# Context of an attention pair in three thirds of 192 queries, one beat behind the moves

## The reference

```python
scores = scale * np.matmul(q, k.transpose(0, 1, 3, 2))
thresh = np.max(scores, axis=-1, keepdims=True) - tau
scores = np.where(scores >= thresh, scores, -1000000000.0)
attn = np.exp(scores - max); attn = attn / (sum(attn) + 1e-09)
x = matmul(attn, v)                     # heads joined: 2304 x 512
h = x @ w_in;  x = (s * relu(h)**2 + b) @ w_out         # layer 0
h = x @ w_in;  x = (h * sigmoid(1.702 * h)) @ w_out     # layer 1
```

## Time and profile before

| | us |
|---|---|
| median of 3 runs (lowest to highest) | 1163.02 (1158.73 to 1167.03) |
| the profiled execution | 1155.08 |
| its span, first to last instruction | 1153.3 |
| TensorE busy | 1050.9 (91%) |
| VectorE busy | 615.6 (53%) |
| GpSimd busy | 782.8 (68%) |
| ScalarE busy | 678.0 (59%) |

### The profile page before, as it was taken

How to read it: one execution, slowest core, us unless ns; L and a number is a source line. 1 busy time by engine, 2 the same in 40 slices (tenths; PEclk the granted TensorE clock), 3 DMA queues, 4 the chain that set the end, 5 groups by cost and what they waited for, 6 DMA issues and landing times.

```text
span 1153.3 us, 18602 instructions
## 1 busy us (share of the span) xinstructions
PE 1050.9 (91%) x6144; PEld 930.8 (81%) x6144; DVE 615.6 (53%) x1556; ACT 678.0 (59%) x1267; POOL 782.8 (68%) x773
## 2 busy tenths in 40 slices
PE   4677547999999999999999999999999999999998
PEld 3565436887888878888898989989999999999997
DVE  6766859998999989897223222232222322222221
ACT  4655436766767677676467666654545545454543
POOL 4655538887878777886476666756676766766673
PEclk9889769999999999999999999999999999999999
DMA  2111177776776767855543443433444434343441
GB/s 96 42 54 53 53 186 201 188 182 178 205 208 179 189 182 198 213 156 153 152 128 117 125 124 120 128 113 125 156 128 146 130 126 155 128 150 126 147 136 65
DMA packets 126623, 162.66 MB, mean 141 GB/s; under 512 B 27328, under 2 KB 68928, under 8 KB 126528
## 3 DMA queue, kind: packets, MB, share of 16 engines
q1 hardware_dynamic: 126528, 161.47, 48.4%
HBM read 124.85 MB, written 4.72 MB: 112 GB/s over the span
## 4 chain that ended last, share of the span: by engine, by line
PE 73%; DVE 9%; SPq 8%; DMA 4%; issue 3%; POOL 2%; ACT 1%; ACTq 0%; DVEq 0%; POOLq 0%
PE y_ps L454 30%; PE scores L436 24%; SPq L282 6%; PE scores L401 5%; PE shared L436 5%; PE scores L349 5%; DVE prob L533 4%; DVE scores L509 4%; DMA prob_t<-blocks 3%; PE shared L401 2%; POOL win_lo L809 1%; SPq L291 1%; PE shared L463 1%; POOL k_lo L789 1%; PE y_ps L371 0%
## 5 line engine op out<-in xcount | busy, mean ns | idle before, releaser
L809 POOL TENSOR_TENSOR win_lo<-raw_in,win_hi 128x512 fp32r<-128x512 f32 x192 | 289.1, 1506 | 97.4 <-ACT win_hi L672 97.4
L816 POOL TENSOR_TENSOR wout_lo<-raw_out,wout_hi 128x512 fp32r<-128x512 f32 x192 | 254.9, 1328 | 100.3 <-ACT wout_hi L679 100.3
L562 DVE TENSOR_TENSOR gate<-scores,gate 128x384 f32<-128x384 f32 x134 | 74.7, 558 | 409.3 <-ACT gate L689 298.5
L454 PE MATMUL y_ps<-wout_hi,g_hi 128*128 128x512 f32 x576 | 227.7, 395 | 0.0
L454 PE MATMUL y_ps<-wout_hi,g_lo 128*128 128x512 f32 x576 | 227.2, 394 | 0.0
L454 PE MATMUL y_ps<-wout_lo,g_hi 128*128 128x512 f32 x576 | 227.2, 394 | 0.0
L640 ACT ACTIVATE prob<-scores,neg_max 128x576 f32<-128x576 f32 (+2 forms) x160 | 118.7, 742 | 144.5 <-DVE scores L509 137.7
L707 ACT CAST g_hi<-gate 128x384 fp32r<-128x384 f32 x192 | 98.6, 514 | 143.5 <-PE y_ps L454 143.2
L436 PE MATMUL scores<-act_hi,win_lo 128*128 128x384 f32 x536 | 180.9, 337 | 0.0
L436 PE MATMUL scores<-act_hi,win_hi 128*128 128x384 f32 x536 | 180.5, 337 | 0.0
L436 PE MATMUL scores<-act_lo,win_hi 128*128 128x384 f32 x536 | 180.0, 336 | 0.0
(11 more groups left out here) (66 smaller groups left out, 1668.1 us busy)
## 6 DMA issues: line engine op xcount, KB each, us to landing
raw_in<-slabs_a SPq DMA_DIRECT2D x96, 256.0 KB, 3.1
raw_out<-slabs_a SPq DMA_DIRECT2D x96, 256.0 KB, 2.8
raw_in<-slabs_b SPq DMA_DIRECT2D x96, 256.0 KB, 2.6
raw_out<-slabs_b SPq DMA_DIRECT2D x96, 256.0 KB, 2.6
qk_raw<-qk SPq DMA_DIRECT2D x32, 576.0 KB, 4.0
prob_t<-blocks SPq DMA_DIRECT2D x144, 100.0 KB, 3.1
prob_t<-blocks SPq DMA_DIRECT2D x144, 80.0 KB, 2.6
v_sb<-v SPq DMA_DIRECT2D x16, 320.0 KB, 3.2
```

What stands on the lines that cost most here:

```text
L454: mm = nc.tensor.matmul(y_ps[g][:], gp[:, n % 2, toks], wp[n % RING_OUT][:], start=(f == 0 and k == 0), stop=(f == SLABS - 1 and k == 2))
L809: nc.gpsimd.tensor_tensor(win_lo[n % RING_IN][:], raw_in[:, n % 2, :], win_hi[n % RING_IN][:].bitcast(F32), ALU.subtract).then_inc(win_lo_ ...
L816: nc.gpsimd.tensor_tensor(wout_lo[n % RING_OUT][:], raw_out[:, n % 2, :], wout_hi[n % RING_OUT][:].bitcast(F32), ALU.subtract).then_inc(wo ...
```

## The change

1. From pair 4 on the context has three pieces of 192 queries in place of four of 160, 160, 160 and 96. They run at beats 5p+8, 5p+9 and 5p+10; beat 5p+7 has none. A piece waits for the moves of every quad that its columns touch.
2. `move_quad` waits for as many pieces of the pair before as its columns overlap: quad 0 for the first, quad 1 for two, quads 2 and 3 for all three. So quad 2 of the first head, issued in beat 5p+5, now waits for the piece that TensorE computes in that same beat. The rule also holds for pair 4, whose moves no longer wait for all of batch 0.
3. In batch 0 `context_hi` comes at the head of the next beat, and `context_lo` right after the first row maximum and limit of that beat.
4. The weight slabs of steps 0 and 1 are loaded at the start of the program in place of beats 26 to 28.

```diff
-PIECES = [(pair, THIRD * n, THIRD, TPH * pair + 7 + n) for pair in range(PAIRS_PER_BATCH) for n in range(3)]
-PIECES += [(pair, RUN * a, QUAD_RUNS[a], TPH * pair + 7 + a)
-           for pair in range(PAIRS_PER_BATCH, PAIRS) for a in range(QUADS)]
+THIRDS = 3
+PIECES = [(pair, THIRD * n, TPH * pair + (7 if pair < PAIRS_PER_BATCH else 8) + n)
+          for pair in range(PAIRS) for n in range(THIRDS)]
...
+def riding(beat):
+    return PIECE_OF[beat] if beat in PIECE_OF and rides(PIECE_OF[beat]) else None
+
+
+def alone(beat):
+    return PIECE_OF[beat] if beat in PIECE_OF and not rides(PIECE_OF[beat]) else None
...
             def move_quad(h, a):
...
-                if h // 2 == PAIRS_PER_BATCH:
-                    sp.wait_ge(context_ready, pieces_of(h // 2))
-                else:
-                    sp.wait_ge(context_ready, pieces_of(h // 2 - 1) + a + 1)
+                sp.wait_ge(context_ready, THIRDS * (h // 2 - 1) + min(a + 1, THIRDS))
...
             def slabs(s):
-                if 0 <= s + 1 < STEPS:
+                if 2 <= s + 1 < STEPS:
                     load_out(s + 1)
-                if 0 <= s + 2 < STEPS:
+                if 2 <= s + 2 < STEPS:
                     load_in(s + 2)
...
+            for n in range(2):
+                load_in(n)
+                load_out(n)
...
             def context_of(piece):
...
                     for side in range(2):
-                        pe.wait_ge(moved[side][q0 // RUN], 64 * (pair - PAIRS_PER_BATCH + 1))
+                        for a in range(q0 // RUN, (q0 + THIRD - 1) // RUN + 1):
+                            pe.wait_ge(moved[side][a], 64 * (pair - PAIRS_PER_BATCH + 1))
...
# VectorE
                     if j < TILES:
                         row_max(j)
                         limit_of(j)
+                    if j % 2 == 0 and alone(beat - 1) is not None:
+                        context_lo(alone(beat - 1))
...
-                if piece_split_in(beat) is not None:
-                    context_lo(piece_split_in(beat))
+                if riding(beat) is not None:
+                    context_lo(riding(beat))
...
# ScalarE
             for beat in range(BEATS):
                 s = beat - MLP_FROM
+                if alone(beat - 1) is not None:
+                    context_hi(alone(beat - 1))
...
-                if piece_split_in(beat) is not None:
-                    context_hi(piece_split_in(beat))
+                if riding(beat) is not None:
+                    context_hi(riding(beat))
```

More of the change, by code:

```diff
@@ L75 @@
 MLP_FROM = 28
-PIECES = [(pair, THIRD * n, THIRD, TPH * pair + 7 + n) for pair in range(PAIRS_PER_BATCH) for n in range(3)]
-PIECES += [(pair, RUN * a, QUAD_RUNS[a], TPH * pair + 7 + a)
-           for pair in range(PAIRS_PER_BATCH, PAIRS) for a in range(QUADS)]
-PIECE_OF = {beat: n for n, (_, _, _, beat) in enumerate(PIECES)}
-BEATS = PIECES[-1][3] + 1
+THIRDS = 3
+PIECES = [(pair, THIRD * n, TPH * pair + (7 if pair < PAIRS_PER_BATCH else 8) + n)
+          for pair in range(PAIRS) for n in range(THIRDS)]
+PIECE_OF = {beat: n for n, (_, _, beat) in enumerate(PIECES)}
+BEATS = PIECES[-1][2] + 1
 FIRST_PURE = BEATS - MLP_FROM
@@ L85, in rides @@
     return PIECES[piece][0] >= PAIRS_PER_BATCH
[L88 to L94, removed]
+def riding(beat):
+    return PIECE_OF[beat] if beat in PIECE_OF and rides(PIECE_OF[beat]) else None
+def alone(beat):
+    return PIECE_OF[beat] if beat in PIECE_OF and not rides(PIECE_OF[beat]) else None
 def pieces_before(beat):
-    return sum(due < beat for _, _, _, due in PIECES)
-def pieces_of(pairs):
-    return sum(pair < pairs for pair, _, _, _ in PIECES)
+    return sum(due < beat for _, _, due in PIECES)
 def act_cols(piece):
-    pair, q0, n, _ = PIECES[piece]
+    pair, q0, _ = PIECES[piece]
     at = (pair // PAIRS_PER_BATCH) * SEQ + q0
-    return pair % PAIRS_PER_BATCH, slice(at, at + n)
+    return pair % PAIRS_PER_BATCH, slice(at, at + THIRD)
 def pieces_for(tile):
@@ L249, in piece_bank @@
         def piece_bank(piece):
-            n = PIECES[piece][2]
-            return scores[1][:, 1, HALF:HALF + n] if rides(piece) else shared[:, 0:n]
+            return scores[1][:, 1, HALF:HALF + THIRD] if rides(piece) else shared[:, 0:THIRD]
         block = ctx.enter_context(nc.Block())
@@ L266, in load_values @@
                 if pair > 0:
-                    sp.wait_ge(context_ready, pieces_of(pair))
+                    sp.wait_ge(context_ready, THIRDS * pair)
                 sp.dma_start(v_sb[:], v[pair]).then_inc(v_loaded, 16)
@@ L323, in _ @@
                     pair = PIECES[PIECE_OF[beat]][0]
-                    if pieces_before(beat + 1) == pieces_of(pair + 1) and pair + 1 < PAIRS:
+                    if pieces_before(beat + 1) == THIRDS * (pair + 1) and pair + 1 < PAIRS:
                         load_values(pair + 1)
@@ L357, in buffer_free @@
                     pe.wait_ge(masked, min(j - 1, TILES))
-                if j % 2 == 1 and pieces_before(j // 2) > pieces_of(PAIRS_PER_BATCH):
+                if j % 2 == 1 and pieces_before(j // 2) > THIRDS * PAIRS_PER_BATCH:
                     pe.wait_ge(context_lo_ready, pieces_before(j // 2))
@@ L401, in context_of @@
                         mm = nc.tensor.matmul(place[64 * side:64 * side + 64, :],
-                                              v_sb[:, side, c, :], prob_t_of(2 * pair + side)[:, c, q0:q0 + n],
+                                              v_sb[:, side, c, :], prob_t_of(2 * pair + side)[:, c, q0:q0 + THIRD],
                                               start=(c == 0), stop=(c == KEY_CHUNKS - 1))
@@ L423, in hidden @@
                 if n == 0:
-                    pe.wait_ge(context_lo_ready, pieces_of(PAIRS_PER_BATCH))
+                    pe.wait_ge(context_lo_ready, THIRDS * PAIRS_PER_BATCH)
                 if n < FIRST_PURE:
@@ L477, in _ @@
                 for j in tiles_of(beat):
-                    if j < TILES or (j % 2 == 1 and beat in PIECE_OF):
+                    if j < TILES or (j % 2 == 1 and riding(beat) is not None):
                         buffer_free(j)
-                    if j % 2 == 1 and beat in PIECE_OF and rides(PIECE_OF[beat]):
-                        context_of(PIECE_OF[beat])
+                    if j % 2 == 1 and riding(beat) is not None:
+                        context_of(riding(beat))
                     if j < TILES:
@@ L485, in _ @@
                         turn_tile(j - 4)
-                if beat in PIECE_OF and not rides(PIECE_OF[beat]):
-                    context_of(PIECE_OF[beat])
+                if alone(beat) is not None:
+                    context_of(alone(beat))
                 mlp(beat - MLP_FROM)
@@ L529, in mask @@
                 dve.wait_ge(exp_ready, j + 1)
-                if j % 2 == 1 and j // 2 in PIECE_OF and rides(PIECE_OF[j // 2]):
-                    dve.wait_ge(context_hi_ready, PIECE_OF[j // 2] + 1)
+                if j % 2 == 1 and riding(j // 2) is not None:
+                    dve.wait_ge(context_hi_ready, riding(j // 2) + 1)
                 p = prob[0:m, j % PROBS, :].rearrange("p (a n) -> p a n", a=2)
@@ L543, in turn @@
                 if t == 0 and h // 2 == PAIRS_PER_BATCH:
-                    dve.wait_ge(context_ready, pieces_of(PAIRS_PER_BATCH - 1))
+                    dve.wait_ge(context_ready, THIRDS * (PAIRS_PER_BATCH - 1))
                 elif t == 0:
@@ L655, in copy_turned @@
                 if t == 0 and h >= 4:
-                    act_eng.wait_ge(context_ready, pieces_of(h // 2 - 1))
+                    act_eng.wait_ge(context_ready, THIRDS * (h // 2 - 1))
                 if t == TPH - 1:
```

## The result

| | before | changed |
|---|---|---|
| median us | 1160.88 (1158.31 to 1167.03, 4 runs) | 1108.45 (1107.61 to 1111.1, 4 runs) |
| ratio to before, 95% interval | | 0.9545 (0.9501 to 0.9589) |
| profiled execution, us | 1155.08 | 1111.1 |
| its span, us | 1153.3 | 1109.3 |

The before column has one run more than the three known when the prediction was made. The medians differ by 52.4 us, the two profiled executions by 44.0. The profiled execution of before was faster than all four of its timed runs, the changed one was the slowest of its four.

A forecast was written before the change was run, and what follows sets the result against it. TensorE was taken to bound the mixed stage, VectorE close behind, with only the first 578 us movable. Gains of 20.2 + 14.0 + 18.7 = 52.9 us gave 1102.2 profiled, 1110 as median; forecast 1100 to 1118, range 1096 to 1128.

The forecast's parts named there:

- the likeliest case: Whole kernel: the three gains come out about as summed, 1100 to 1118 us, chance 0.58.
- Part A: Batch 0, beats 7 to 22: the earlier split removes TensorE's waits for `context_lo`, gain 20.2 us.
- rival 1: Batch 0: TensorE's clock stays at the lower level, up to 10 us less gain, 1120 us, chance 0.12.
- Part B: Transition to moves, beats 23 to 27: 5 beats take 27.5 us in place of 41.5, gain 14.0 us.
- The loads at the start: Four slabs loaded at the program's start: counted at 0, with bounds of 1 us of loss and 1 us of gain.
- Part C: Mixed stage: a pair takes 33.8 us, without a wait for moves; gain 1.7 us a pair, 18.7 for 11 waits.
- rival 3: Mixed stage: SyncE's new wait delays the loads behind it, each of 11 pairs loses 7 us, 1187 us, chance 0.03.
- The wait added on SyncE: Beat 5p+5: SyncE stands at quad 2 for the third piece; nothing else waits, 1.3 us to spare.
- Rivals 2 and 4: Rival 2: mixed stage gives nothing, as VectorE bounds it or moves wait anew; 18 us less, 1128, chance 0.12.
- rival 4: Batch 0: the wait for `context_lo` becomes one for transposes, norms or masks; half the gain, 1122 us, chance 0.06.

The follow-up runs named there:

- the square above: Four runs, all with the early split, compared in beats 26 and 27: the wait on thirds clears beat 26, the later context clears beat 27.
- thirds without the beat: The changed kernel with the thirds of pairs 4 to 15 one beat earlier, in beats 5p+7 to 5p+9: 1160.98 us, ratio 0.9980.
- the run with one early load: The changed kernel with the next w_out slab's load issued between the two quads in beat 5p+6 only: 1108.86 us, ratio 0.9551.

## Why the prediction was right, step by step

**The time.** 1110 was forecast, 1108.45 measured, by the likeliest case. Part of that nearness is luck: on the profiled execution I forecast 1102.2 and it was 1111.1, because the sum gave 52.9 us and the stages gave 44. The median moved by 52.4, because the runs of before lay 6 us above their profiled one and those of the changed kernel 3 us below theirs. The record shows where most of the 6 us lie. In the 30 executions of the kernel before whose granted clock is known (profiled one included) it is 0.967 to 0.975, and time goes with it: 1170.6 us at 0.967, 1162.2 to 1165.8 at 0.969, 1155.1 to 1160.1 at 0.974. The profiled execution had 0.974. The eight of the changed kernel had 0.983 to 0.986, in 1107.6 to 1111.1 us. So part of the gain in the medians is TensorE's clock, which rises when the waits go; the 3 us on the changed side it does not explain (0.984 and 0.985 in all four runs).

**Part A, 20.2 forecast, 17.7 measured.** The mechanism held: in beats 7 to 21 no wait for `act_lo` is left, and the context beats are 4.15 and 4.7 us (4.3 forecast). The sign "no wait of L401 for `act_lo` before 150 us" failed by two waits, 3.0 us in all. They are in beats 23 and 24, where the `turn` on VectorE holds up the subtraction; I had let these two waits go like the other six. Over 15 beats it is 63.9 us in the four executions with an early split and no slow beat among them, 65.5 in this one, against 61.8: the 9 beats that had no wait before took 3.8 to 5.0 us (beat 21, where `turn` sets in, is one of them), not 4.0 each. The 1.6 us more here are one context beat at the lower clock (5.71 us, beat 7). Of 12 contexts in batch 0, 6 were stretched to 2.7 us and more before and 2 after. The granted clock of beats 7 to 21 rose from 0.92 to 0.97. So rival 1 happened in small: its case was 10 us, about 2 came. The Trainium skill, page TensorE: Matmul & The Clock Gate, section "HAM oscillation — how this bites in real kernels", says that idle gaps of TensorE bring the lower clock back. The trace agrees in direction: with the 2.5 us waits gone the clock mostly stayed up, although gaps of 1.5 to 1.7 us remain in each pair.

**Part B, 14.0 forecast, 15.3 measured.** The beats came out as summed (4.99 to 5.70 us), the `turn` just fits (SyncE's chain ran 124.08 to 134.78 and the `turn` at 132.80 needs its first half only), and the square above shows the two causes. The first feed-forward matmul came at 142.42 us, not near 138, because beat 7 began 1.7 us later than before and part A gave 2.5 less. The loads at the start cost and bring nothing that the runs can tell, as counted.

**Part C, 18.7 forecast, 12.9 measured; the term that was mis-sized.** TensorE's beats were right: an undisturbed pair takes 32.84 us, and their sum was 32.8. Wrong was what I put on top, 0.7 for row transposes and 0.3 because VectorE "needs its 33.6".

VectorE's 33.6 us were busy time in a window of 36 us, longer than a pair. In the pair of beats 57 to 61 alone it is 32.3 us busy of 35.26 before and 31.6 of 32.84 after. It does not bound the pair, and an undisturbed pair gains 2.4 us, more than the 1.7 forecast.

The row changes are the mis-sized term. They cost 1.5 us a pair (34.33 on average against 32.84), not 0.7, because the two pairs that hold them lost 1.7 and 2.7 us where I let every pair gain. In beat 47 the wait for moves had probably covered the row copies (1.56 us of wait there before, 2.25 us for the rows' bank now); no run separates that. Beat 63 lost 3.3 us to the late slab and the clock behind it. I had looked at the late slabs (rival 3) only as a loss in every pair and priced the queue for its own users, the moves; the wait came out on ScalarE, and cost time only where the row copy stands behind it.

The starting figure was off too. The period of 35.48 us ends in beat 82, and beats 80 to 82 have no score tiles; over whole pairs it was 35.66. And the stretch won is 51 beats long, 10.2 pairs and not 11.

**The wait added on SyncE.** Right as forecast: the moves' users do not wait, and the slack is thin. With the second quad 0.5 us later (one more load between) waits of 0.4 to 4.0 us appeared. Rival 3 did not come. With one beat more of hold its mechanism does, and the kernel is 1.4% slower than before. But its price of a beat of 7 us in each of 11 pairs was too high: beats 28 to 78 of that run are 24 us longer than before, not 77.

**Rivals 2 and 4.** Neither: the mixed stage gave 12.9 of 18.7 us, and the 22.7 us of waits in batch 0 turned into 3.0 for the same wait. TensorE's wait for masks, the place that rival 4 names, stayed at 28.3 us against 27.4.

## What to carry to other kernels

A wait moved off the engine that bounds the kernel lands in the queue of the engine that issues; price not only what is queued behind it but what is queued behind *those* on the engines that they feed. Distance in the schedule and the size of a piece have to be chosen together: over beats 28 to 78 each alone lost (32 and 24 us), and both together won 12.9. When a stall is removed, ask which other work ran under it. And read a window of whole periods before calling an engine the next bound.

## What the runs showed of the hardware

- Issue time sets the moves' pace: 8 DMAs take SyncE 5.25 us, 0.65 us each, while one lands 2.1 to 3.1 us after issue (medians by size, 48 to 100 KB). The Trainium skill, page DMA: Bandwidth & Descriptors, section "Issuing engines are not separate DMA queues", calls the time to initiate a DMA usually small relative to the DMA itself. For one move that is so here, about a quarter of the time to landing. But the landings overlap and the issues do not, so for a chain of 8 the issues are the larger part.
- A wait of TensorE can cost more than its length. Behind 2.9 to 3.4 us of waiting, context pieces of 1.85 us took 3.3 to 3.5 us in 5 of 11 pairs (thirds without the beat), and behind 3.38 us in beat 63 the granted clock was 0.57 for the next 4 us; behind 1.71 us it stayed at 1.00.
- Which of the first beats TensorE runs at 1.2 GHz differs between executions of one kernel: beat 7 lasted 5.71 us in one profile of the changed kernel and 4.13 in the other, and in the run with one early load it was beat 12.
